# Splitting the first transfers of a fused retention-and-MLP kernel over two queues, and reordering its first Strassen-like unit

## The reference

```python
gamma = 1.0 - 2.0 ** (-5.0 - np.arange(H))
for t in range(S):
    state = gamma * state + einsum('bhd,bhe->bhde', k[:, :, t], v[:, :, t])
    y[:, :, t] = scale * einsum('bhd,bhde->bhe', q[:, :, t], state)
x = y as (1536 tokens, 512)
h = x @ w_in                       # 512 x 2048
x = (h * sigmoid(1.702 * h)) @ w_out
xn = x / sqrt(mean(x * x) + 1e-6) * rms_g
g, val = xn @ w_gate, xn @ w_val   # 512 x 1536 each
out = (g * sigmoid(g) * val) @ w_out2
```

## Time and profile before

| | |
|---|---|
| median of three executions | 583.98 us |
| the profiled execution, its own time | 583.44 us |
| its span | 581.6 us |
| TensorE busy, matmul | 573.3 us (99%) |
| VectorE busy | 359.2 us (62%) |
| ScalarE busy | 298.1 us (51%) |
| GpSimd busy | 172.1 us (30%) |
| moved by DMA | 52.84 MB |

### The profile page before, as it was taken

The page is one execution under the profiler, slowest core; times in us unless marked ns, Lnnn a source line. Parts: engine busy times, 40 slices in busy tenths (PEclk is TensorE's granted clock), DMA queues, the critical chain, the costliest instruction groups (busy, mean ns, idle before and its releaser), DMA issues.

```text
span 581.6 us, 9400 instructions
## 1 busy us (share of the span) xinstructions
PE 573.3 (99%) x3640; PEld 551.8 (95%) x3640; DVE 359.2 (62%) x486; ACT 298.1 (51%) x501; POOL 172.1 (30%) x222
## 2 busy tenths in 40 slices
PE   7999999999999999999999999999999999999997
PEld 7988999999999999999999999998889999998886
DVE  5797555676425667775346768678755666666432
ACT  1244766645336766645237655574444555564321
POOL 2386444000222452000314464410051545420000
PEclk9999999999999999999999999999999999999999
DMA  8981222322112222312202222233213322224202
GB/s 319 392 292 37 74 72 73 108 73 73 38 36 73 72 74 70 111 39 72 73 0 74 73 74 72 74 84 99 73 36 125 93 73 73 73 74 112 69 1 108
DMA packets 24220, 52.84 MB, mean 91 GB/s; under 512 B 1776, under 2 KB 1904, under 8 KB 24176
## 3 DMA queue, kind: packets, MB, share of 16 engines
q1 hardware_dynamic: 23600, 50.41, 28.2%
q10 hardware_dynamic: 576, 1.84, 0.8%
HBM read 49.09 MB, written 3.15 MB: 90 GB/s over the span
## 4 chain that ended last, share of the span: by engine, by line
PE 97%; DVE 1%; DMA 1%; issue 0%; ACT 0%
PE bank L539 20%; PE twin L539 20%; PE twin L480 11%; PE twin L483 11%; PE twin L482 11%; PE bank L483 6%; PE bank L480 6%; PE bank L482 6%; PE twin L392 2%; PE bank L438 2%; PE bank L425 1%; DMA arena<-attn_in 1%; PE bank L409 1%; DVE x_lo L787 0%; PE bank L580 0%
## 5 line engine op out<-in xcount | busy, mean ns | idle before, releaser
L778 DVE TENSOR_TENSOR w_lo<-raw,w_hi 128x512 fp32r<-128x512 f32 (+2 forms) x148 | 149.3, 1024 | 49.7 <-ACT w_hi L612 49.5
L1059 POOL TENSOR_TENSOR raw<-raw 128x256 f32<-128x256 f32 x40 | 32.1, 803 | 317.1 <-DMA raw<-w 312.5
L480 PE MATMUL twin<-x_hi,w_hi 128*128 128x384 f32 x360 | 120.5, 335 | 0.6 <-ACT arena L676 0.6
L483 PE MATMUL twin<-x_hi,w_lo 128*128 128x384 f32 x360 | 120.3, 334 | 0.0
L482 PE MATMUL twin<-x_lo,w_hi 128*128 128x384 f32 x360 | 120.2, 334 | 0.0
L612 ACT ACTIVATE w_hi<-raw 128x512 fp32r<-128x512 f32 (+2 forms) x148 | 109.0, 763 | 18.0 <-PE bank L539 7.6
L813 DVE TENSOR_TENSOR g_lo<-arena,g_hi 128x768 fp32r<-128x768 f32 x56 | 54.3, 970 | 74.8 <-ACT g_hi L642 74.8
L642 ACT ACTIVATE g_hi<-arena 128x768 fp32r<-128x768 f32 x56 | 47.5, 848 | 103.6 <-PE bank L539 103.6
L480 PEld LDWEIGHTS twin<-x_hi,w_hi 128*128 128x128 f32 x360 | 67.6, 188 | 0.9 <-ACT arena L676 0.9
L482 PEld LDWEIGHTS twin<-x_lo,w_hi 128*128 128x128 f32 x360 | 67.6, 188 | 0.0
L483 PEld LDWEIGHTS twin<-x_hi,w_lo 128*128 128x128 f32 x360 | 67.6, 188 | 0.0
(11 more groups left out here) (105 smaller groups left out, 995.9 us busy)
## 6 DMA issues: line engine op xcount, KB each, us to landing
raw<-w SPq DMA_DIRECT2D x68, 512.0 KB, 3.7
arena<-attn_in SPq DMA_DIRECT2D x22, 512.0 KB, 7.9
out<-x SPq DMA_DIRECT2D x1, 1536.0 KB, 8.6
out<-x SPq DMA_DIRECT2D x6, 256.0 KB, 2.0
arena<-attn_in ACTq DMA_DIRECT2D x2, 512.0 KB, 10.1
arena<-tables ACTq DMA_DIRECT2D x1, 512.0 KB, 6.1
arena<-tables ACTq DMA_DIRECT2D x1, 256.0 KB, 9.8
ident<-ident_in SPq DMA_DIRECT2D x1, 64.0 KB, 12.8
```

The source lines that it names most:

```text
L480: pe.matmul(dst, w_hi[q][:, w], x_hi[:, x], start=start and kk == 0, stop=False, skip_group_check=True)
L483: mm = pe.matmul(dst, w_lo[q][:, w], x_hi[:, x], start=False, stop=kk == 1, skip_group_check=True)
L778: dve.tensor_tensor(w_lo[q % 3][:, dst], src, w_hi[q % 3][:, dst].bitcast(F32), ALU.subtract)\
L1059: pool.tensor_tensor(s1, a21, a22, ALU.add).then_inc(w_sums, 1)
```

## The change

It has three parts.

- **First transfers.** Q and K of steps 0 and 1, the mask, and K and V of step 0 are each split into two halves of 256 KB with 2 KB per partition; SyncE's queue takes one half, ScalarE's the other. Q and K of both steps now stand ahead of the mask. Waits on them ask for both halves (`qk_at`, `kv_at`). SyncE issues two transfers more at the start and ScalarE two more.
- **TensorE's start and VectorE's.** Two products of ones stand between `scores(0)` and `scores(1)` and four behind `scores(1)` (before: three and none). `new_products(0)` moves behind `from_chunk(0)`, so the fifth K and V load, which overwrites slot 0, gets a second wait, on `kv_done`. VectorE masks steps 0 and 1 one after the other, ahead of `decay_q(1)` and `new_state(0)`.
- **Unit 0.** M6 moves ahead of M3, so M3 stands between M6 and M7. VectorE forms the low part of T2 first, then that of T3, then that of the last third of the unit's weights (before: weights, T3, T2).

```diff
-FILL = 3
+FILL = (2, 4)
-LOWER = {True: (B11, B21, T1, B22, T3, T2, T4), False: (B11, B21, T1, T2, B22, T3, T4)}
+LOWER = {True: (B11, B21, T1, B22, T2, T3, T4), False: (B11, B21, T1, T2, B22, T3, T4)}
...
+        def qk_at(a):
+            return 16 * (a // SLOTS) + (32 if a % SLOTS < 2 else 16)
+        def kv_at(a):
+            return 16 * (a // SLOTS) + (32 if a % SLOTS == 0 else 16)
...
-            load(0)
-            load(1)
+            for a in range(2):
+                sp.dma_start(slot[a][:, 0:512], attn_in[BATCH * a, :, 0:512]).then_inc(qk_in[a], 16)
+            sp.dma_start(mask[:, 0:512], tables[:, T_MASK:T_MASK + 512]).then_inc(mask_in, 16)
+            sp.dma_start(slot[0][:, 1536:2048], attn_in[0, :, 1536:2048]).then_inc(kv_in[0], 16)
             load_kv(1)
             load(2)
...
                     sp.wait_ge(y_done, b - SLOTS + 1)
+                    if b == SLOTS:
+                        sp.wait_ge(kv_done, 1)
                     load_kv(b)
...
             for a in range(0, STEPS, 2):
                 scores(a)
                 if a == 0:
-                    for _ in range(FILL):
-                        pe.matmul(gate[1][:, 0:P], ones[:, :], ones[:, :], start=True, stop=True)
+                    fill(FILL[0])
                 scores(a + 1)
                 if a == 0:
-                    new_products(0)
+                    fill(FILL[1])
                     from_state(0)
                     from_chunk(0)
+                    new_products(0)
                     from_state(1)
                     new_products(1)
...
                     pe.wait_ge(w_lo_done, lo_at[r] + 2)
+                    product(6, n, 2, 1, 2, T2, False)
                     pe.wait_ge(m5_copied, n + 1)
                     product(3, n, 1, 1, 3, B22, False)
-                    product(6, n, 2, 1, 2, T2, False)
...
-            act.dma_start(mask, tables[:, T_MASK:T_Q]).then_inc(mask_in, 16)
-            act.dma_start(slot[0][:, 1024:2048], attn_in[0, :, 1024:2048]).then_inc(kv_in[0], 16)
+            for a in range(2):
+                act.dma_start(slot[a][:, 512:1024], attn_in[BATCH * a, :, 512:1024]).then_inc(qk_in[a], 16)
+            act.dma_start(mask[:, 512:1024], tables[:, T_MASK + 512:T_Q]).then_inc(mask_in, 16)
+            act.dma_start(slot[0][:, 1024:1536], attn_in[0, :, 1024:1536]).then_inc(kv_in[0], 16)
             act.dma_start(q_table, tables[:, T_Q:T_ALL]).then_inc(q_table_in, 16)
...
                 masked(a)
+                masked(a + 1)
                 if a == 0:
                     decay_q(1)
                     new_state(0)
-                masked(a + 1)
...
                 if a == 10:
                     sum_x(0, T2)
+                    lower_x(0, T2)
+                    lower_x(0, T3)
                     lower_w(0, 2)
-                    lower_x(0, T3)
-                    lower_x(0, T2)
```

More of the change, by code:

```diff
@@ L385, in scores @@
                 q, k = slot[r][:, 0:512], slot[r][:, 512:1024]
-                pe.wait_ge(qk_in[r], 16 * (a // SLOTS) + 16)
+                pe.wait_ge(qk_in[r], qk_at(a))
                 if a >= 2:
@@ L402, in new_products @@
                 v = slot[r][:, 1536:2048]
-                pe.wait_ge(kv_in[r], 16 * (a // SLOTS) + 16)
+                pe.wait_ge(kv_in[r], kv_at(a))
                 pe.wait_ge(k_decayed, m + 1)
@@ L432, in from_chunk @@
                 v = slot[a % SLOTS][:, 1536:2048]
-                if a % CHUNKS == CHUNKS - 1:
-                    pe.wait_ge(kv_in[a % SLOTS], 16 * (a // SLOTS) + 16)
+                pe.wait_ge(kv_in[a % SLOTS], kv_at(a))
                 pe.wait_ge(probs_done, a + 1)
@@ L444, in _, with fill @@
             pe.wait_ge(ones_set, 1)
-            for _ in range(WARM_UP):
-                pe.matmul(gate[1][:, 0:P], ones[:, :], ones[:, :], start=True, stop=True)
+            def fill(count):
+                for _ in range(count):
+                    pe.matmul(gate[1][:, 0:P], ones[:, :], ones[:, :], start=True, stop=True)
+            fill(WARM_UP)
             for a in range(0, STEPS, 2):
@@ L885, in _ @@
             dve.wait_ge(factors_set, 2)
-            dve.wait_ge(mask_in, 16)
+            dve.wait_ge(mask_in, 32)
             shape = [P, LEAVES, PAIRS, 2]
@@ L918, in decay_q @@
                     dve.wait_ge(q_table_in, 16)
-                dve.wait_ge(qk_in[r], 16 * (a // SLOTS) + 16)
+                dve.wait_ge(qk_in[r], qk_at(a))
                 if x >= 2:
@@ L1039, in decay_k @@
                 r, m = a % SLOTS, state_at(a)
-                pool.wait_ge(kv_in[r], 16 * (a // SLOTS) + 16)
+                pool.wait_ge(kv_in[r], kv_at(a))
                 if m >= 2:
@@ L1048, in decay_q @@
                 r, x = a % SLOTS, cross_at(a)
-                pool.wait_ge(qk_in[r], 16 * (a // SLOTS) + 16)
+                pool.wait_ge(qk_in[r], qk_at(a))
                 if x >= 2:
```

## The result

The changed kernel takes 585.48 us (median of 13 runs, 584.34 to 586.60), the kernel before, run beside it, 583.98 us. The ratio is 1.0025, 95% interval 1.0016 to 1.0033: 1.5 us slower, between 0.9 and 1.9. The forecast was 583.8 us with a range up to 584.8, so the result lies outside the range. The profiled execution took 585.48 us with a span of 583.6 us, 2.0 us over the profiled execution of before.

What follows compares the result with a forecast made beforehand. TensorE was taken to bound the kernel, through the time of unit 1's first matmul. Terms 0 - 0.85 + 0.65 gave -0.2 us from the median of 583.98, so 583.8 us, with a range of 582.4 to 584.8.

Steps and rivals of the forecast that it cites:

- What bounds the kernel: TensorE, busy 99% of the span; a shift of unit 1's first matmul (57.79 us) reaches the end unchanged.
- Term 1: Start and attention: 0 us, no early lead survives the line of transfers; bounds -1.3 us, or slower if halves move slower.
- half rows are slow: Rival, first transfers: 2 KB rows delay every later arrival, 0.8 us at 350 GB/s, 1.9 at 297; say 585.0 us; chance 0.12.
- The lead of `scores(0)`: Start: `scores(0)` at 5.4 us instead of 6.73, 1.3 us earlier, with nothing of it surviving to the end.
- Three more ones at the low clock: Start, TensorE: six products of ones instead of three cost below 1 us if the wait for `decay_q(1)` does not cover them.
- Term 2: Unit 0, TensorE: M3 between M6 and M7 removes the wait for M6's copy, -0.85 us.
- Term 3: Unit 0, other engines: unit 1 waits for its weights' low part until 57.5 us, +0.65 us; bounds 0 and +1.45.
- The chain of turns: Unit 0: VectorE and GpSimd take turns on a shared port pair, delaying the low part of unit 1's weights to 57.45 us.
- one turn more: Unit 0, upper bound +1.45 us: GpSimd gets an extra turn, 0.6 us for it and 0.2 for the order behind.

Runs made afterwards that it cites:

- dma_only: Kernel before with only the first transfers in halves over both queues in the new order, with their waits: 584.99 us, ratio 1.0012.
- split_aligned: `dma_only` with the table array padded so that mask and Q table rows begin at multiples of 512 bytes: 585.16 us, ratio 1.0014.
- same_queue: Kernel before with the same first transfers cut in halves, each half on its old queue in its old place: 585.26 us, ratio 1.0017.
- whole_order: Kernel before with whole 4 KB-row transfers, Q and K of step 1 moved ahead of the mask: 584.37 us, ratio 1.0002.
- eng_only: Kernel before with only the change's second part, the new order of TensorE and VectorE at the start; transfers as before: 584.59 us, ratio 1.0005.
- swap_aligned: `u0_swap` with the table array padded so that mask and Q table rows begin at multiples of 512 bytes: 583.40 us, ratio 0.9984.
- u0_swap: Kernel before with only M6 moved ahead of M3 in unit 0, VectorE's order kept: 583.43 us, ratio 0.9981.
- more_ones: Changed kernel with ten more products of ones ahead of `from_state(0)`: 586.32 us, ratio 1.0033 to the kernel before.
- u0_whole: Kernel before with the change's third part alone, M6 ahead of M3 and VectorE's new order: 584.60 us, ratio 1.0000.

## Why the prediction was wrong

- **What bounds the kernel: right.** All of the difference lies ahead of unit 1's first matmul; no later wait appeared.
- **Term 1 (0) is the first step that failed.** I took the halves to move at the rate of whole transfers, because the weights' 2 KB rows moved 414 GB/s at 52 us. In that stretch one queue moved one kind of transfer. At the start, halves of all four kinds of transfer took 49 to 52 us of engine time per MB in place of 44, and the three kernels that differ from the one before in their first transfers alone (`dma_only`, `split_aligned` with its padded table, `same_queue`) lie 0.7 to 1.0 us above it. The rival "half rows are slow" named the slower transfers and the place, K of step 4, 0.6 us late in this pair of traces and 0.9 on average over all; its chance of 0.12 was too small, its 350 GB/s and 0.8 us nearly the measured size. In its place, Term 1 should have been +0.7 to +1.0.
- **The rest of the reasoning on the start held in part.** The lead of `scores(0)`, even at 1.85 us, did not survive; the order alone (`whole_order`) and the engines' part (`eng_only`) gave nothing that could be measured. But `decay_q(1)`, which was to stay at 11.50 us, came at 12.78; TensorE did not idle longer ahead of `new_products(4)`, it came there last; and the sum has no term for the clock, which fell in the trace and whose share is open. Three more ones at the low clock were put below 1 us; in `eng_only` two took 1.22 us from 7.88 us on, at a granted clock of 0.90 falling to 0.50. No term rests on that.
- **Term 2 (-0.85): right.** The swap alone made unit 0 0.86 us shorter and the kernel 1.1 us faster.
- **Term 3 (+0.65) was mis-sized: it measured +1.2.** The chain of turns was right link by link. Its start was taken from one trace, in which VectorE had a lead of 2.29 us. With the lead of 1.63 us in the changed kernel's trace the same working gives 7.85 us, against 7.75 measured. It also had the copy of M6 done ahead of M7, which waited 0.43 us for it here. The bound of +1.45, "one turn more", did hold the value, but for another cause.
- **The sum:** 0.85 at the start (between 0.7 and 1.0), -0.85 and +1.2 give +1.2 us; the kernels show +1.5 (0.9 to 1.9). The two traces show +1.9 at unit 1's start. Single traces of kernels whose start is alike differ by as much: unit 0 begins at 51.09 us in `swap_aligned` and at 52.71 in `u0_swap`, whose medians are 583.40 and 583.43 us. So the 1.7 us by which step 10's decay came later are not all the change's; the medians tell its size.

## What to carry to other kernels

The transfers stood in a saturated line here, and a split that looked free was paid for by what stood behind it: compare DMA engine time per MB in the stretch that you change, not the rate of a lone one, and try the new order with whole transfers first. When an instruction is put ahead of others on an engine because its consumer moved forward, ask what it waits for itself: here the low part of T2 waited 0.9 us for ScalarE, the old order already had it in time, and the move of M6 alone kept its whole gain. A chain without slack must be costed from the worst lead that its first engine may have, not from the one in the trace at hand.

## What was not expected of the hardware

- The first transfers cut in two, with 2 KB rows in place of 4 KB, took 11 to 16% more DMA engine time per byte at the start of the program (49.3 and 51.5 us per MB against 44.4), with both halves on one queue or one on each. A lone 512 KB transfer with 2 KB rows showed no such price (41 us per MB).
- TensorE's clock fell to the lower level behind the 1.93 us of idling that ended at 10.83 us, and behind 1.97 us that ended at 10.82 us in `whole_order`; holding it up gained no time at the end (`more_ones`).
- The time at which K and V of step 10 arrive moves by up to 2 us between traces (its decay starts at 42.45 us in `u0_whole` and at 44.36 in `u0_swap`, which issue the same transfers), while the 523.9 us from unit 1 to the end are the same to 0.1 us.
